# The first tiles of a chunked linear attention: where VectorE forms the next decayed r, and which queue brings the third raw tile

## The reference

```python
for t in range(S):
    kt, vt, rt = (k[:, :, t], v[:, :, t], r[:, :, t])
    cur = np.einsum('bhd,bhe->bhde', u[None] * kt, vt)
    y[:, :, t] = np.einsum('bhd,bhde->bhe', rt, state + cur)
    state = w[None, :, :, None] * state + np.einsum('bhd,bhe->bhde', kt, vt)
```

## Time and profile before

| | us |
|---|---|
| median of 3 timed executions | 304.85 (304.63, 304.85, 309.64) |
| profiled execution, its own time | 307.98 |
| span of its trace (first to last instruction) | 306.2 |
| mean granted TensorE clock, share of full speed | 0.993 |
| PE busy | 292.7 (96% of the span) |
| DVE busy | 178.4 (58%) |
| POOL busy | 64.5 (21%) |
| ACT busy | 85.4 (28%) |

### The profile page before, as it was taken

One profiled execution on the slowest core, in us unless ns is written; L12 is line 12 of the kernel. 1 busy time (PEld: TensorE's weight loads), 2 busy tenths in 40 slices (PEclk: granted clock), 3 DMA queues, 4 the chain that ended last, 5 costly groups with the idle time before them and its releaser, 6 DMA issues.

```text
span 306.2 us, 8794 instructions
## 1 busy us (share of the span) xinstructions
PE 292.7 (96%) x3230; PEld 243.1 (79%) x3231; DVE 178.4 (58%) x411; ACT 85.4 (28%) x181; POOL 64.5 (21%) x103
## 2 busy tenths in 40 slices
PE   7898999979999999999999999999999999999993
PEld 7787888768888877744654878999989999999992
DVE  4799888956979797546332687343352523525232
ACT  1122313123132231612311776222222222222220
POOL 1589546524555340200000010000000000000000
PEclk9999999989999999999999999999999999999999
DMA  6999999976678969999999559902020020200202
GB/s 156 263 249 278 275 275 246 245 241 199 193 240 277 280 208 396 389 430 424 428 356 362 192 183 382 361 4 103 0 103 0 0 103 0 103 0 0 103 0 103
DMA packets 31312, 62.39 MB, mean 204 GB/s; under 512 B 4912, under 2 KB 22960, under 8 KB 30256
## 3 DMA queue, kind: packets, MB, share of 16 engines
q1 hardware_dynamic: 27824, 56.70, 56.0%
q10 hardware_dynamic: 3456, 5.25, 6.8%
HBM read 52.49 MB, written 9.44 MB: 202 GB/s over the span
## 4 chain that ended last, share of the span: by engine, by line
PE 89%; DVE 2%; issue 2%; SPq 2%; DMA 2%; ACT 1%; DVEq 0%
PE ps L1500 12%; PE ps L1501 11%; PE ps L1502 11%; PE ps L1229 8%; PE ps L1171 8%; PE ps L1252 4%; PE ps L1191 4%; PE ps L1511 4%; PE ps L1260 4%; PE ps L1379 3%; PE ps L1398 3%; PE ps L1241 3%; PE ps L1205 3%; DMA raw<-rT 2%; PE ps L1478 2%
## 5 line engine op out<-in xcount | busy, mean ns | idle before, releaser
L889 DVE SCALAR_TENSOR_TENSOR h_lo<-ps,h_hi 128x512 fp32r<-128x512 f32 x48 | 32.7, 690 | 65.4 <-ACT h_hi L1080 65.4
L1500 PE MATMUL ps<-w_hi,h_hi 128*128 128x384 f32 x192 | 65.4, 341 | 0.9 <-issue 0.4
L1501 PE MATMUL ps<-w_lo,h_hi 128*128 128x384 f32 x192 | 64.5, 336 | 0.0
L1502 PE MATMUL ps<-w_hi,h_lo 128*128 128x384 f32 x192 | 64.3, 335 | 0.0
L1080 ACT ACTIVATE h_hi<-ps 128x512 fp32r<-128x512 f32 x48 | 28.2, 598 | 80.6 <-PE ps L1511 74.6
L595 POOL TENSOR_TENSOR kt<-raw,dec_k 128x512 f32<-128x512 f32 x23 | 36.3, 1579 | 41.4 <-PE ps L1171 26.9
L1500 PEld LDWEIGHTS ps<-w_hi,h_hi 128*128 128x128 f32 x192 | 36.0, 188 | 5.2 <-issue 3.5
L1501 PEld LDWEIGHTS ps<-w_lo,h_hi 128*128 128x128 f32 x192 | 36.0, 188 | 1.3
L1502 PEld LDWEIGHTS ps<-w_hi,h_lo 128*128 128x128 f32 x192 | 36.1, 188 | 0.0
L1171 PE MATMUL ps<-rt,kt 48*128 48x128 f32 x384 | 28.8, 288 | 3.3 <-issue 2.6
L725 DVE TENSOR_TENSOR at<-ps,mask 128x1024 f32<-128x1024 f32 x24 | 29.3, 1220 | 3.3 <-PE ps L1171 3.3
(11 more groups left out here) (188 smaller groups left out, 374.3 us busy)
## 6 DMA issues: line engine op xcount, KB each, us to landing
w_first<-w1a SPq DMA_DIRECT2D x8, 768.0 KB, 7.3
w_first<-w2a SPq DMA_DIRECT2D x8, 768.0 KB, 6.5
a_slot<-w1a SPq DMA_DIRECT2D x4, 1536.0 KB, 14.7
x_slot<-w2a SPq DMA_DIRECT2D x3, 1536.0 KB, 14.0
out<-x SPq DMA_DIRECT2D x1, 4608.0 KB, 14.8
out<-x SPq DMA_DIRECT2D x24, 192.0 KB, 1.9
kn<-k_nat SPq DMA_DIRECT2D x20, 192.0 KB, 5.8
vn<-v_nat SPq DMA_DIRECT2D x20, 192.0 KB, 5.9
```

Of the source, the lines that this page charges most:

```text
L889: dve.scalar_tensor_tensor(out=h_lo[f % HB][:], in0=bank[4 + f % HB], scalar=0.0, in1=h_hi[f % HB][:].bitcast(F32), op0=ALU.max, op1=ALU.s ...
L1500: pe.matmul(bank[t][:, 0:DM], hh, w2_hi[:, f, :], start=(f == 0), stop=False)
L1501: pe.matmul(bank[t][:, 0:DM], hh, w2_lo[:, f, :], start=False, stop=False)
L1502: last = pe.matmul(bank[t][:, 0:DM], hl, w2_hi[:, f, :], start=False, stop=(f == FT - 1))
```

## The change

Three edits.

1. For the tiles 0, 1 and 2, DVE forms rt of the next tile behind the mask and behind rk, where it did so ahead of the mask. From tile 3 on the order is the old one.
2. ACT issues raw2 (four DMAs) right behind raw0, ahead of the loads of v. SP issues raw3 where it issued raw2.
3. The load of v for tile 0 goes from ACT to SP, ahead of k by token of tile 0.

```diff
-    RL_REP, KEEP = 12, 8
+    RL_REP, KEEP, EARLY_R = 12, 8, 3
...
+            sp.dma_start(vn[0][:, 0:DM], v_nat[0, 0]).then_inc(v_in[0], 16)
             load_nat(0)
-            first_raw(sp, 2)
+            first_raw(sp, 3)
             load_nat(1)
-            first_raw(sp, 3)
             load_nat(2)
             load_nat(3)
...
-                if n + 1 < NCHUNK * B:
+                if EARLY_R <= n < NCHUNK * B - 1:
                     decayed_r(n + 1)
...
                 dve.tensor_tensor(rk[:], r_raw[b], k_raw[b], ALU.mult).then_inc(rk_ready, 1)
+                if n < EARLY_R:
+                    decayed_r(n + 1)
...
             first_raw(act, 0)
-            for n in range(NV):
+            first_raw(act, 2)
+            for n in range(1, NV):
                 act.dma_start(vn[n][:, 0:DM], v_nat[0, n]).then_inc(v_in[n], 16)
```

## The result

| | before | changed |
|---|---|---|
| median, us | 305.33 (304.63 to 309.64, 4 executions) | 310.21 (308.24 to 313.85, 4 executions) |
| ratio, 95% interval | | 1.0133 (1.0084 to 1.0182) |
| span of the profiled execution | 306.2 | 307.9 |

The changed kernel is slower, by 4.0 us on this measurement. Two later comparisons of the same kernel, with more executions, gave 1.0078 (1.0041 to 1.0114, 12 executions) and 1.0124 (1.0065 to 1.0183, 6 executions): the three together say about 3 us. The forecast of 306.8 had the direction, but its range ended at 308.6. Of the four executions of the changed kernel the one with a mean granted clock of 0.998 took 308.24; the other three had 0.990, 0.985 and 0.979 and took 309.73, 310.69 and 313.85.

The account below looks back on a forecast made before the run. PE, busy 96% of the span, was taken as the bound. 0.70 at tile 1, 0.51 at tile 2, -0.08 at tile 3 and 0.19 + 0.73 of holding gave +2.0: 304.85 + 2.0 = 306.8 us, range 304.5 to 308.6.

Parts of the forecast that it names:

- The bound: PE's own sequence sets the time; rt behind mask and rk delays the scores of tile 1 by 0.70 us.
- POOL and DVE hold each other up: Tiles 2 and 3: a POOL product and a two-operand DVE product block each other, adding 0.19 + 0.73 us.
- ks of tile 1 comes with kn1 at 17.1, waits for rt: On POOL, ks of tile 1 arrives after rt of tile 2 has started, waits and runs 17.5 to 18.5.
- The first rival: POOL slips in between rk and rt, holding rt of tile 2 or 3: +3.0 to +3.3 us, 308.0; chance 0.20.
- The term that was put at nothing: The profiled execution's stall and clock loss, about 3.5 us, were left out of the median: 304.85 + 2.0.
- The clock: Rival: new PE idle times ahead of tiles 1 to 3 halve TensorE's clock, price 1.7 us, 308.5; chance 0.08.
- Nothing behind gives it back.: From tile 3 on PE's order carries the delay on, since PE has no waits there to absorb it.
- the rival that gave it 0.12 and 0.8 us: Delay partly given back: one PE "issue" stall doesn't come, 0.8 us off, 305.2 to 306.0; chance 0.12.
- 0.3 us at most: Ceiling of the gain: PE's 0.17 us idle from 12.96 to 20.07, plus a little ahead of 16.22.
- Not slower: Rival: raw tiles land later in timed executions, where the new order doesn't wait at rt; at best 304.5; chance 0.10.
- the edits to the queues costing nothing: Edits 2 and 3: same bytes reordered; v of tile 0, ACT's extra issues and SP's earlier load were put as covered or nothing.

Follow-up runs that it names:

- e3: The changed kernel with one wait added: POOL's ks of tiles 0, 1 and 2 waits for rt of the tile behind it; 1.0065 of the kernel before.
- e12: The kernel before with edits 2 and 3 and POOL paced (kt waits for rt, ks for rk of the same tile in early tiles); ratio 0.9935 (0.9902 to 0.9968).
- e9: The kernel before with POOL paced: kt of tiles 2 to 8 waits for rt, ks of tiles 1 to 7 for rk of the same tile; ratio 0.9989.
- e2: Edits 2 and 3 alone on the kernel before, rt ahead of the mask as before; ratio 1.0011 (0.9981 to 1.0042).

## Why the prediction was wrong

- **The bound** (PE's sequence; rt in the chain to the scores). Right. Tile 1 lost 0.74 against 0.70 forecast.
- **POOL and DVE hold each other up.** Right, and confirmed by e3. In the Trainium skill, SBUF — State Buffer, section "Who interferes with whom", it is stated that the order of issue decides who blocks; the traces agree: ks queued at 15.97 ran ahead of rt, which wanted to start at 16.45.
- **The step that failed first** is the choice between two orders of arrival: "ks of tile 1 comes with kn1 at 17.1, waits for rt". It came at 15.97, and raw of tile 4 by 19.99 instead of 21.5, so POOL slipped in at both places. Tile 2 was 2.08 late instead of 1.40 and tile 3 3.51 (13.69 against 10.18) instead of 2.05. The first rival had this with 3.0 to 3.3 us. It was given 0.20 with margins of 0.1 to 0.3 us, but in kernels with the same queues kn of tile 0 came at anything from 12.2 to 14.3 and kn of tile 1 from 15.8 to 17.4. Margins that small against such scatter leave an even chance at best. In all three profiles of the changed kernel kn of tile 1 came before 16.87 (15.97 to 16.39).
- **The term that was put at nothing.** That step alone does not carry the time out of the range: the rival's time is 308.0, and the 2.56 that was left at tile 6 makes 307.9 with the median of 305.33. The forecast took the stall and the clock loss of the earlier trace rows out of the kernel before and gave the changed kernel none. Its first profile has both at the same place (1.23 idle ahead of 68.12, half the clock for 3.4 us; from tile 12 to tile 13 it is 7.89, where a kernel without the stall, e12, has 4.70). In both profiles the stall falls inside one score product, behind 5 of its 16 matmuls, so it is no wait for an operand; what it is is open. Three of the four first executions had clocks of 0.990 or less. These losses are the likely rest of the 4.0 to 4.9 us; how they share it is open. The larger samples had medians 3.2 and 2.7 above the kernel before (308.75 and 308.52), so it is in part luck that the first four lay so high.
- **The clock.** Named as a rival with 0.08 and 1.7 us, for the three idle times of the first tiles. There it came in one of three profiles and cost 1.55. More than half of the executions had a low mean clock, but no record says that they lost it there. The argument against it (one idle time of 0.72 cost nothing) took a single gap for three in a row.
- **"Nothing behind gives it back."** Wrong: 3.51 at tile 3 is 2.56 at tile 6, and 2.6 at the last tile of the attention with the stalls from tile 12 to 13 left out. That is the rival that gave it 0.12 and 0.8 us. The kernel before has a slow tile 5 (5.59 us), in which POOL's arrears meet rt and rk and PE stands for 0.81 with no semaphore named (it started at 29.82, behind an x product of DVE that ended at 29.78, so this "issue" was very likely a wait for DVE too, where the prediction read that PE is not held by data); the changed kernel, whose POOL caught up while PE waited, has 4.70 there.
- **"0.3 us at most" could be gained.** Too narrow: it looked at the stretch to 20.07 only. With POOL paced and the new queues the time is 2.0 us less (e12), with POOL paced alone there is no difference that can be measured (e9).
- **Not slower** (late raw tiles) and the edits to the queues costing nothing: the first did not happen, the second held (e2).

## What to carry to other kernels

A product that is moved to just behind another one on the same engine also moves into a row of operations that a neighbour can break into; ask not only what it waits for but who else can take the turn between the two. Where an outcome hangs on whether a DMA lands before or behind some product by a few tenths of a us, give both outcomes like chances and let the range hold both. A wait that makes the helper engine keep step with the busy one, and so costs the helper idle time that it has anyway, can be worth more than moving the busy engine's own work. And a mean over an execution, such as the granted clock, says that something was lost and not where: look for the stretch in a profile before a gap is blamed for it.

## What the runs showed of the hardware

- rt and rk (two operands in SBUF) took 0.67 to 0.69 alone and up to 1.76 beside a POOL product; the mask (one operand in SBUF, one in PSUM) stayed at 1.21 to 1.23 in every kernel, also beside kt.
- Three idle times of TensorE of 0.67, 1.34 and 1.6 us within 10.5 us were followed by a fall of the granted clock to half in one of the two profiles that had them, and not in the other. Single idle times of 1.78 ahead of 66.37 (kernel before) and 1.23 ahead of 68.12 (changed kernel) were followed by one as well.
- The landing of one and the same DMA moved by 1.6 to 2.1 us between kernels that issue it at the same place of the queue (kn of tile 1 and of tile 0), and by 0.4 to 0.6 us between the three profiles of the changed kernel.
